# Attention slot order and TensorE wait placement in a fused attention and two-MLP kernel

## The chip, the core and the metric

The kernel runs on one core of a Trainium2 chip (trn2). The metric is the device time of one execution in microseconds, the median of three runs for the kernel before: 488.89 us (487.48 to 489.02). Engines are named as the profile names them: PE is TensorE (PEld its weight loads), DVE is VectorE, ACT is ScalarE, POOL is GpSimd, SP is the engine that issues the DMAs.

## The reference

Three stages follow one another: a local attention with block summaries, an MLP with a squared ReLU, and a second MLP whose hidden layer is a softmax-gated unit with a layer norm. Cut to what matters:

```python
# attention, B=2 H=8 S=768 D=64, block 32, window 16
k_sum = k.reshape(B, H, nb, block, D).max(axis=3)
v_sum = v.reshape(B, H, nb, block, D).mean(axis=3)
scores_l = where(|i - j| < window, scale * q @ k.T, -1e9)
scores_s = scale * q @ k_sum.T + log(block)
a = softmax(concat([scores_l, scores_s]))
x = a @ concat([v, v_sum])              # then (1536 tokens, 512)
# first MLP, 512 -> 2048 -> 512
h = maximum(x @ w_in, 0)
y = h * h @ w_out
# second MLP, 512 -> 1024 -> 512
h = y @ w_in
solu = h * softmax(h)
ln = (solu - mean(solu)) / sqrt(var(solu) + 1e-6) * g_ln
out = ln @ w_out
```

## The kernel before

Every large product is done in three matmuls, since each operand is split into a rounded part and the rest (`PASSES`: high x high, high x low, low x high). The attention is cut into 32 units `u`. A unit is a pair of heads and 192 query rows, three tiles of 64 rows, and has three parts on PE: `scores(u)` (L825, 64x64 tiles with 120 moving columns), `turned(u)` (L844, three transposes of the normalised probabilities) and `values(u)` (L874, 120 rows by 64 columns). Between scores and turned lie the eviction with mask and the maximum on DVE (`maxima`), the exponentials on ACT (`exps`) and the normalisation on DVE (`reciprocals`, `normalise`). Between turned and values ACT copies the result to SBUF (`copy_probsT`), and after values ACT makes `x_hi` (`x_high`) and DVE `x_lo` (`x_low`).

The first eight units run in the ramp. The other 24 are woven into the first MLP, which runs over four chunks of 384 tokens and 16 hidden tiles each: `up(n)` (L897, twelve 128x384 matmuls) and `down(n)` (L927, twelve more) alternate, two half steps per `n`. The table `SLOTS` says before which half step an attention slot stands and which units it handles: values of `a`, scores of `a + 2`, turned of `a + 1`. Slots are three half steps apart in the first chunk and four later. For units from 8 on, one PSUM bank pair serves all three: scores lie in bank 0, the transposed probabilities and the values' result in bank 1, where the result also reaches into the end of bank 0. `slot_ahead` puts waits that a coming slot needs on matmuls of the half step before it.

The second MLP goes over 12 tiles of 128 tokens. Step `s` on PE is: 24 matmuls of 512 columns for the hidden layer of tile `s` (L1022), eight transposes of the centred tile `s - 1` (L1037), and 24 matmuls for the output of tile `s - 2` (L1049). At `s = 0` and `s = 1` there is no output yet. On DVE a tile goes through its maximum (L774), `solu` (L782), `cen` (L789), and then the low part of the transposed tile before it, `lnT_lo` (L795). All engines run their own lists in the order of the code and meet at semaphores.

## Time and profile before

| what | before |
|---|---|
| median of three runs | 488.89 us (487.48 to 489.02) |
| the profiled execution | 488.89 us, its span 487.0 us |
| PE busy | 478.3 us, 98% of the span |
| DVE, ACT, POOL busy | 254.5, 207.6, 30.5 us |
| chain that ended last, by engine | PE 90%, DMA 3%, DVE 3%, SP 2%, ACT 1% |
| PE lines in the chain | L927 27%, L897 27%, L1049 12%, L1022 12%, L825 4%, L874 3%, L844 3%, L1037 2% |

The page gives one profiled execution. Its first part is the busy time of each engine; the chain is followed back from the last instruction to what released it, step by step. Matmuls are pipelined and their ends are modelled, so their records overlap: the distance between two starts is the time one took of the engine. A timeline row joins neighbouring instructions of one line, with the first start, the time from there to the last end, and their count. For values and scores each matmul has two records, so x12 stands for six. The granted clock is given as a share of full speed.

### The profile page before, as it was taken

What the parts mean: (1) busy time and instruction counts of PE and PEld (TensorE: products, weight loads), DVE (VectorE), ACT (ScalarE), POOL (GpSimd) and SP (SyncE); (2) the same over time, 40 slices, a digit from 0 to 9 for tenths busy, and PEclk for the clock granted to TensorE, in tenths of its full rate; (3) what the DMA queues carried; (4) which work ended last, traced back from release to release, by engine and by line L of the source; (5) the groups of instructions that cost most, each with busy time, mean ns of one, the idle gap of its engine ahead of it and who ended that gap; (6) DMA issues with size and microseconds to landing.
All of it is one profiled execution on the core that took longest, in us unless ns stands there. A gap on an engine that the chain in (4) does not pass through costs nothing.

```text
span 487.0 us, 8121 instructions
## 1 busy us (share of the span) xinstructions
PE 478.3 (98%) x3134; PEld 435.6 (89%) x3134; DVE 254.5 (52%) x511; ACT 207.6 (43%) x525; POOL 30.5 (6%) x62
## 2 busy tenths in 40 slices
PE   7899999999999999999999999999999999999997
PEld 5778999999999999999999999999888888888885
DVE  3779768886544444644443344446574444444440
ACT  2787665654343333533343333334353333333341
POOL 2421000211000000000000000000000000000000
PEclk9999999999999999999999999999999999999999
DMA  8999332121400010400000412121122000000001
GB/s 306 287 326 320 103 108 87 55 74 29 155 22 22 21 36 27 145 27 22 22 1 1 131 44 79 52 62 70 44 86 66 22 23 22 26 34 28 22 22 44
DMA packets 26823, 37.39 MB, mean 77 GB/s; under 512 B 2496, under 2 KB 16736, under 8 KB 26784
## 3 DMA queue, kind: packets, MB, share of 16 engines
q1 hardware_dynamic: 26784, 36.86, 24.2%
q8 instruction: 25, 0.41, 0.4%
q14 instruction: 14, 0.11, 0.1%
HBM read 30.41 MB, written 6.29 MB: 75 GB/s over the span
## 4 chain that ended last, share of the span: by engine, by line
PE 90%; DMA 3%; DVE 3%; SPq 2%; ACT 1%; issue 1%; ACTq 0%; DVEq 0%
PE bank L927 27%; PE bank L897 27%; PE bank L1049 12%; PE bank L1022 12%; PE bank L825 4%; DMA v_first<-vrows 3%; PE bank L874 3%; PE bank L844 3%; PE bank L1037 2%; DVE solu L782 1%; DVE stat L774 1%; DVE lnT_lo L795 0%; SPq L259 0%; SPq L250 0%; DVE cen L789 0%
## 5 line engine op out<-in xcount | busy, mean ns | idle before, releaser
L897 PE MATMUL bank<-x_hi,win_hi 128*128 128x384 f32 x256 | 87.9, 343 | 0.0
L927 PE MATMUL bank<-h_hi,wout_hi 128*128 128x384 f32 x256 | 86.0, 336 | 0.0
L897 PE MATMUL bank<-x_hi,win_lo 128*128 128x384 f32 x256 | 85.7, 335 | 0.0
L927 PE MATMUL bank<-h_hi,wout_lo 128*128 128x384 f32 x256 | 85.7, 335 | 0.0
L897 PE MATMUL bank<-x_lo,win_hi 128*128 128x384 f32 x256 | 85.7, 335 | 0.0
L927 PE MATMUL bank<-h_lo,wout_hi 128*128 128x384 f32 x256 | 85.6, 334 | 0.0
L651 DVE TENSOR_TENSOR sqr<-relu 128x384 f32<-128x384 f32 x64 | 35.9, 561 | 88.2 <-ACT relu L491 87.4
L491 ACT ACTIVATE relu<-bank 128x384 f32<-128x384 f32 x64 | 31.5, 491 | 108.9 <-PE bank L897 108.9
L897 PEld LDWEIGHTS bank<-x_hi,win_hi 128*128 128x128 f32 x256 | 48.1, 188 | 0.3 <-issue 0.2
L897 PEld LDWEIGHTS bank<-x_lo,win_hi 128*128 128x128 f32 x256 | 48.2, 188 | 0.0
L927 PEld LDWEIGHTS bank<-h_lo,wout_hi 128*128 128x128 f32 x256 | 48.1, 188 | 0.0
L927 PEld LDWEIGHTS bank<-h_hi,wout_hi 128*128 128x128 f32 x256 | 48.1, 188 | 0.0
L897 PEld LDWEIGHTS bank<-x_hi,win_lo 128*128 128x128 f32 x256 | 48.1, 188 | 0.0
L927 PEld LDWEIGHTS bank<-h_hi,wout_lo 128*128 128x128 f32 x256 | 48.1, 188 | 0.0
L774 DVE TENSOR_REDUCE stat<-bank 128x1 f32<-128x1024 f32 x12 | 14.7, 1225 | 49.1 <-PE bank L1022 49.1
L442 ACT ACTIVATE probs<-probs,neg_max 128x120 f32<-128x120 f32 x96 | 36.5, 382 | 8.7 <-DVE neg_max L624 8.6
L569 ACT ACTIVATE e_sb<-bank,stat 128x1024 f32<-128x1024 f32 x12 | 13.4, 1116 | 61.3 <-DVE stat L774 61.3
L1049 PE MATMUL bank<-win_hi,lnT_hi 128*128 128x512 f32 x96 | 38.4, 400 | 0.0
L655 DVE TENSOR_TENSOR h_lo<-sqr,h_hi 128x384 fp32r<-128x384 f32 x64 | 35.8, 559 | 4.3
L1049 PE MATMUL bank<-win_hi,lnT_lo 128*128 128x512 f32 x96 | 37.5, 391 | 0.0
L1049 PE MATMUL bank<-win_lo,lnT_hi 128*128 128x512 f32 x96 | 37.4, 390 | 0.0
L451 ACT COPY probsT<-bank 120x384 f32<-120x384 f32 x32 | 15.3, 478 | 48.0 <-PE bank L844 47.6
(79 smaller groups left out, 721.5 us busy)
## 6 DMA issues: line engine op xcount, KB each, us to landing
win_raw<-w_in_t SPq DMA_DIRECT2D x8, 512.0 KB, 12.8
wout_raw<-w_out_t SPq DMA_DIRECT2D x8, 512.0 KB, 14.1
win_raw<-w_t SPq DMA_DIRECT2D x8, 512.0 KB, 3.3
v_ext<-vwin SPq DMA_DIRECT2D x24, 144.0 KB, 3.2
k_raw<-kT SPq DMA_DIRECT2D x8, 400.0 KB, 4.1
out<-o_sb SPq DMA_DIRECT2D x12, 256.0 KB, 2.0
q_sb<-qT SPq DMA_DIRECT2D x24, 96.0 KB, 2.8
v_first<-vrows SPq DMA_DIRECT2D x4, 384.0 KB, 11.0
```

The lines of the kernel that those rows point to most:

```text
L442: last = nc.scalar.activation(probs[:, s, c], probs[:, s, c], ACT.Exp, bias=neg_max[:, s, t:t + 1], accum_out=row_sum[:, s, t:t + 1])
L451: nc.scalar.copy(probsT[0:KX, u % 2, :], src).then_inc(probsT_ok, 1)
L491: nc.scalar.activation(relu[:, n % 2, :], up_bank(n), ACT.Relu).then_inc(relu_ok, 1)
L651: nc.vector.tensor_tensor(sqr[:, n % 3, :], relu[:, n % 2, :], relu[:, n % 2, :], ALU.mult)\
L655: nc.vector.tensor_tensor(h_lo[:, n % 3, :], sqr[:, n % 3, :], h_hi[:, n % 3, :].bitcast(F32), ALU.subtract).then_inc(hlo_ok, 1)
L774: nc.vector.tensor_reduce(stat[:, p, 0:1], h2_bank(s), AX.X, ALU.max, negate=True).then_inc(m2_ok, 1)
L825: last = nc.tensor.matmul(out_[e * QT:(e + 1) * QT, t * KX:(t + 1) * KX], q_tile(u, rows, t), k_ext[rows, p, t * KX:(t + 1) * KX], start=T ...
L844: last = nc.tensor.transpose(turned_bank(u, t), probs[:, u % 2, t * KX:(t + 1) * KX], ident[:, 0:P])
L897: last = nc.tensor.matmul(up_bank(n), win[a][:, f * WC + k * P:f * WC + (k + 1) * P], x[b][:, c % 2, k * CH:(k + 1) * CH], start=(k == 0 a ...
L927: last = nc.tensor.matmul(down_bank(d), wout[a][:, f * WC + d * P:f * WC + (d + 1) * P], h[b][:, n % 3, :], start=(f == 0 and a == 0 and b ...
L1022: last = nc.tensor.matmul(bank[:, (0, 6)[p] + half, :], y_tile(s, a, k), w2[b][:, (k * FH + half) * WC:(k * FH + half + 1) * WC], start=(k ...
L1049: last = nc.tensor.matmul(bank[:, 4 + p, :], ln[a][:, p, f * P:(f + 1) * P], w2[b][:, (F2 + f) * WC:(F2 + f + 1) * WC], start=(f == 0 and ...
```

## The change

The change has two parts.

1. In a slot of the MLP loop, PE now issues values of `a`, then turned of `b`, then scores of `c`; scores and turned have changed places. PSUM is laid out anew for it: two of the transposed tiles lie in bank 1, the third in bank 0 behind the scores, and the values' result in bank 1 alone. ACT copies the transposed probabilities in two pieces, `copy_probsT` for two tiles and `copy_last` for the third, which waits until DVE has evicted the new scores. `x_high` loses its wait for that eviction and stands between the two copies. The wait for `q` moves from a matmul of the half step before to the second transpose.
2. In the second MLP, waits that stood in front of the transposes (L1037), of the output matmuls (L1049) and of the next hidden layer (L1022) now stand on matmuls in the middle of the stream before them. The waits for `cen`, `lnT_lo` and `o` are on the 16th, 19th and 22nd of the 24 matmuls of the hidden layer, those for `solu` and `y` on two of the last output matmuls.

```diff
@@ -213,12 +212,10 @@
         def turned_bank(u, t):
             if u < UPC:
                 return bank[0:KX, 1 + 2 * (u % 2), t * P:(t + 1) * P]
-            return bank[0:KX, 1, P + t * P:P + (t + 1) * P]
-
-        later_bank = bank[:, 0:2, :].rearrange("p b c -> p (b c)")
+            return bank[0:KX, 1, t * P:(t + 1) * P] if t < TPU - 1 else bank[0:KX, 0, UC:UC + P]
 
         def xT_bank(u):
-            return bank[:, 4 + u % 2, 0:UQ] if u < UPC else later_bank[:, WC - QT:WC - QT + UQ]
+            return bank[:, 4 + u % 2, 0:UQ] if u < UPC else bank[:, 1, 2 * P:2 * P + UQ]
 
         def mean_bank(p):
             return bank[0:NB, 6 + p % 2, 0:P]
@@ -447,15 +444,20 @@
                 act.wait_ge(probsT_ps, u + 1)
                 if u >= 2:
                     act.wait_ge(attn_ps, u - 1)
-                src = bank[0:KX, 1 + 2 * (u % 2), 0:TPU * P] if u < UPC else bank[0:KX, 1, P:P + TPU * P]
-                nc.scalar.copy(probsT[0:KX, u % 2, :], src).then_inc(probsT_ok, 1)
+                if u < UPC:
+                    nc.scalar.copy(probsT[0:KX, u % 2, :], bank[0:KX, 1 + 2 * (u % 2), 0:TPU * P])\
+                      .then_inc(probsT_ok, 1)
+                else:
+                    nc.scalar.copy(probsT[0:KX, u % 2, 0:2 * P], bank[0:KX, 1, 0:2 * P])
+
+            def copy_last(u):
+                act.wait_ge(masked_ok, min(u + 2, UNITS))
+                nc.scalar.copy(probsT[0:KX, u % 2, 2 * P:3 * P], turned_bank(u, 2)).then_inc(probsT_ok, 1)
 
             def x_high(u):
                 slot, cols = x_cols(u)
                 act.wait_ge(attn_ps, u + 1)
                 if u >= UPC:
-
-                    act.wait_ge(masked_ok, min(u + 3, UNITS))
                     act.wait_ge(probsT_ps, min(u + 2, UNITS))
                 if u >= 2 * UPC:
                     act.wait_ge(y_saved[u % PPB], 32 * (u // UPC - 1))
@@ -536,6 +538,7 @@
             hidden(1)
             copy_probsT(8)
             w_in_high(3)
+            copy_last(8)
             exps(9)
             w_out_high(1)
             for n in range(STEPS):
@@ -548,6 +551,8 @@
                         copy_probsT(SLOTS[h][1])
                     if h in X_AT:
                         x_high(X_AT[h])
+                    if h in SLOTS and SLOTS[h][1] is not None:
+                        copy_last(SLOTS[h][1])
                 for h in (2 * n, 2 * n + 1):
                     if h in SLOTS and SLOTS[h][2] is not None:
                         exps(SLOTS[h][2])
@@ -812,7 +817,7 @@
                     pe.wait_ge(qf_in[min(u, 2)], 16)
                 if u % UPB < PPB:
                     pe.wait_ge(kbc_ok, (u // UPB) * PPB + p + 1)
-                if u in (UPC, UPC + 1):
+                if u == UPC:
                     queries(u)
                 if 2 <= u <= UPC:
                     pe.wait_ge(masked_ok, u - 1)
@@ -841,6 +846,8 @@
                     pe.wait_ge(probsT_ok, u)
                 pe.wait_ge(norm_ok, u + 1)
                 for t in range(TPU):
+                    if t == 1 and UPC < u + 1 < UNITS:
+                        queries(u + 1)
                     last = nc.tensor.transpose(turned_bank(u, t), probs[:, u % 2, t * KX:(t + 1) * KX], ident[:, 0:P])
                 last.then_inc(probsT_ps, 1)
 
@@ -864,7 +871,6 @@
                         pe.wait_ge(xlo_ok, u - 1)
                 elif u == UPC:
                     pe.wait_ge(vkept_ok, 1)
-                    pe.wait_ge(masked_ok, UPC + 2)
                 elif UPB <= u < UPB + PPB:
                     pe.wait_ge(vs_in[p], 16)
                 pe.wait_ge(probsT_ok, u + 1)
@@ -880,9 +886,7 @@
             def slot_ahead(h, k):
 
                 if h + 1 in SLOTS:
-                    u, _, c = SLOTS[h + 1]
-                    if k == 1 and c is not None:
-                        queries(c)
+                    u = SLOTS[h + 1][0]
                     if k == 2:
                         pe.wait_ge(vw_in[u % PPB], 16 * (u // PPB - HPC + 1))
                     if k == 3:
@@ -982,10 +986,10 @@
                     if j in SLOTS:
                         a, b, c = SLOTS[j]
                         values(a)
+                        if b is not None:
+                            turned(b)
                         if c is not None:
                             scores(c)
-                        if b is not None:
-                            turned(b)
                     if j % 2 == 0:
                         up(n + 2)
                     else:
@@ -999,6 +1003,17 @@
                     return (y_hi, y_lo)[a][:, i % 2, k * P:(k + 1) * P]
                 at = k * CH + (i % TPC) * P
                 return x[a][:, (i // TPC) % 2, at:at + P]
+
+            def h2_ahead(s):
+
+                if s >= 2:
+                    pe.wait_ge(solu_ok, s - 1)
+
+            def y_ahead(s):
+                if s < (NCHUNK - 2) * TPC:
+                    pe.wait_ge(y_in[s % 2], 32 * (s // 2 + 1))
+                else:
+                    pe.wait_ge(yclo_ok, KD * (s // TPC + 1))
 
             for s in range(TT + 2):
                 p = s % 2
@@ -1010,14 +1025,18 @@
                         pe.wait_ge(xlo_ok, UNITS)
                     if s == 1:
                         pe.wait_ge(relu_ok, STEPS)
-                    if s >= 2:
-                        pe.wait_ge(solu_ok, s - 1)
-                    if s < (NCHUNK - 2) * TPC:
-                        pe.wait_ge(y_in[p], 32 * (s // 2 + 1))
-                    else:
-                        pe.wait_ge(yclo_ok, KD * (s // TPC + 1))
+                    if s < 3:
+                        h2_ahead(s)
+                        y_ahead(s)
                     for half in range(FH):
                         for k in range(KD):
+
+                            if half == 1 and k == 1 and s >= 2:
+                                pe.wait_ge(cen_ok, s)
+                            if half == 1 and k == 2 and s >= 2:
+                                pe.wait_ge(lnlo_ok, s - 1)
+                            if half == 1 and k == 3 and s >= 4:
+                                pe.wait_ge(o_ok, s - 3)
                             for a, b in PASSES:
                                 last = nc.tensor.matmul(bank[:, (0, 6)[p] + half, :], y_tile(s, a, k),
                                                         w2[b][:, (k * FH + half) * WC:(k * FH + half + 1) * WC],
@@ -1028,10 +1047,11 @@
                     down(STEPS - 2)
                     down(STEPS - 1)
                 if 1 <= s <= TT:
-                    pe.wait_ge(cen_ok, s)
                     if s == 1:
+                        pe.wait_ge(cen_ok, s)
                         pe.wait_ge(yclo_ok, KD * (NCHUNK - 1) + 2)
-                    else:
+                    elif s == TT:
+                        pe.wait_ge(cen_ok, s)
                         pe.wait_ge(lnlo_ok, s - 1)
                     for f in range(F2):
                         last = nc.tensor.transpose(bank[:, 2 + f // 4, (f % 4) * P:(f % 4 + 1) * P],
@@ -1041,10 +1061,16 @@
                     if s == 2:
                         pe.wait_ge(w2_lo_ok, F1)
                         pe.wait_ge(yclo_ok, KD * NCHUNK)
-                    if s >= 4:
+                    if s >= TT:
                         pe.wait_ge(o_ok, s - 3)
-                    pe.wait_ge(lnlo_ok, s - 1)
+                    if s == TT + 1:
+                        pe.wait_ge(lnlo_ok, s - 1)
                     for f in range(F2):
+
+                        if f == F2 - 2 and s + 1 < TT:
+                            h2_ahead(s + 1)
+                        if f == F2 - 1 and s + 1 < TT:
+                            y_ahead(s + 1)
                         for a, b in PASSES:
                             last = nc.tensor.matmul(bank[:, 4 + p, :], ln[a][:, p, f * P:(f + 1) * P],
                                                     w2[b][:, (F2 + f) * WC:(F2 + f + 1) * WC],
```

PE, a slot of the first chunk (unit 11 as `a`), before: values, scores, turned, and the first matmul of `down`.

```order
156 L874 MATMUL bank<-probsT,v_ext 64x64 [waits probsT_ok]
157 L874 MATMUL bank<-probsT,v_ext 64x64 x5
158 L825 MATMUL bank<-k_ext,q_sb 64x120 [waits kwin_ok]
159 L825 MATMUL bank<-k_ext,q_sb 64x120 x5
160 L844 MATMUL bank<-ident,probs 120x128 [waits norm_ok]
161 L844 MATMUL bank<-ident,probs 120x128 x2
162 L927 MATMUL bank<-h_hi,wout_hi 128x384 [waits hlo_ok,wout_lo_ok]
```

The same slot in the changed kernel, whose lines are numbered a little differently (L880 values, L851 turned, L830 scores, L931 down).

```order
158 L880 MATMUL bank<-probsT,v_ext 64x64 [waits probsT_ok]
159 L880 MATMUL bank<-probsT,v_ext 64x64 x5
160 L851 MATMUL bank<-ident,probs 120x128 [waits norm_ok]
161 L851 MATMUL bank<-ident,probs 120x128 [waits q_in3]
162 L851 MATMUL bank<-ident,probs 120x128
163 L830 MATMUL bank<-k_ext,q_sb 64x120 [waits kwin_ok]
164 L830 MATMUL bank<-k_ext,q_sb 64x120 x5
165 L931 MATMUL bank<-h_hi,wout_hi 128x384 [waits hlo_ok,wout_lo_ok]
```

The transposes now stand between values and scores, and scores stand next to the large matmuls.

PE, second MLP at `s = 2`, before: the last nine matmuls of the hidden layer and what follows them.

```order
1805 L1022 MATMUL bank<-win_hi,y_hi 128x512
1806 L1022 MATMUL bank<-win_lo,y_hi 128x512
1807 L1022 MATMUL bank<-win_hi,y_lo 128x512
1808 L1022 MATMUL bank<-win_hi,y_hi 128x512
1809 L1022 MATMUL bank<-win_lo,y_hi 128x512
1810 L1022 MATMUL bank<-win_hi,y_lo 128x512
1811 L1022 MATMUL bank<-win_hi,y_hi 128x512
1812 L1022 MATMUL bank<-win_lo,y_hi 128x512
1813 L1022 MATMUL bank<-win_hi,y_lo 128x512
1814 L1037 MATMUL bank<-ident,cen 128x128 [waits lnlo_ok,cen_ok]
1815 L1037 MATMUL bank<-ident,cen 128x128 x7
1816 L1049 MATMUL bank<-win_hi,lnT_hi 128x512 [waits lnlo_ok,yclo_ok,w2_lo_ok]
```

The same place in the changed kernel (L1041, L1057 and L1075 there).

```order
1828 L1041 MATMUL bank<-win_hi,y_hi 128x512 [waits cen_ok]
1829 L1041 MATMUL bank<-win_lo,y_hi 128x512
1830 L1041 MATMUL bank<-win_hi,y_lo 128x512
1831 L1041 MATMUL bank<-win_hi,y_hi 128x512 [waits lnlo_ok]
1832 L1041 MATMUL bank<-win_lo,y_hi 128x512
1833 L1041 MATMUL bank<-win_hi,y_lo 128x512
1834 L1041 MATMUL bank<-win_hi,y_hi 128x512
1835 L1041 MATMUL bank<-win_lo,y_hi 128x512
1836 L1041 MATMUL bank<-win_hi,y_lo 128x512
1837 L1057 MATMUL bank<-ident,cen 128x128 x8
1838 L1075 MATMUL bank<-win_hi,lnT_hi 128x512 [waits yclo_ok,w2_lo_ok]
```

The two waits of the transposes have moved nine and six matmuls ahead.

## Rows read from the trace of the kernel before

**Rows 1.** The page: span, PE's busy time, the chain's shares by engine.
```profile
span 487.0 us, 8121 instructions
...
PE 478.3 (98%) x3134; PEld 435.6 (89%) x3134; DVE 254.5 (52%) x511; ACT 207.6 (43%) x525; POOL 30.5 (6%) x62
...
PE 90%; DMA 3%; DVE 3%; SPq 2%; ACT 1%; issue 1%; ACTq 0%; DVEq 0%
```

**Rows 2.** Stretches: length, busy of each engine, PEclk, DMA share, GB/s.
```profile
105.00:280.00 175.00, 175.00 (x1265) 167.68 (x1264) 83.10 (x176) 68.91 (x201) 7.09 (x16) 1.00 0.15 46
```

**Rows 3.** Waits of PE, the longest: total us, times, longest us.
```profile
PE bank L825 <- DMA q_first<-q_head: 1.7, 1, 1.7
```

**Rows 4.** Timeline of PE, a slot of the first chunk: start, us, instruction.
```profile
67.22 0.57 PE L874 MATMUL bank<-probsT,v_ext 120*64 120x64 f32 x12
67.72 0.83 PE L825 MATMUL bank<-k_ext,q_sb 64*64 64x120 f32 x12
68.48 0.54 PE L844 MATMUL bank<-ident,probs 128*120 128x128 f32 x3
68.78 0.42 PE L927 MATMUL bank<-h_hi,wout_hi 128*128 128x384 f32 x1
69.04 0.34 PE L927 MATMUL bank<-h_lo,wout_hi 128*128 128x384 f32 x1
```

**Rows 5.** Timeline of PE, the last two slots, which have no scores.
```profile
260.60 0.57 PE L874 MATMUL bank<-probsT,v_ext 120*64 120x64 f32 x12
261.10 0.54 PE L844 MATMUL bank<-ident,probs 128*120 128x128 f32 x3
...
270.42 0.45 PE L897 MATMUL bank<-x_hi,win_hi 128*128 128x384 f32 x1
270.70 0.34 PE L897 MATMUL bank<-x_lo,win_hi 128*128 128x384 f32 x1
```

**Rows 6.** Timeline of PE in the ramp: transposes, then scores.
```profile
23.30 0.55 PE L844 MATMUL bank<-ident,probs 128*120 128x128 f32 x3
23.78 0.83 PE L825 MATMUL bank<-k_ext,q_first 64*64 64x120 f32 x12
```

**Rows 7.** Timeline of PE, the one place where scores stand before large matmuls.
```profile
38.12 0.83 PE L825 MATMUL bank<-k_ext,q_sb 64*64 64x120 f32 x12
38.88 0.44 PE L897 MATMUL bank<-x_hi,win_hi 128*128 128x384 f32 x1
39.16 0.33 PE L897 MATMUL bank<-x_lo,win_hi 128*128 128x384 f32 x1
```

**Rows 8.** Timeline of PE's weight loads at the same place.
```profile
38.88 0.19 PEld L897 LDWEIGHTS bank<-x_hi,win_hi 128*128 128x128 f32 x1 [0.16 <-issue]
```

**Rows 9.** The chain: twelve matmuls behind scores, and twelve behind transposes.
```profile
38.95 2.30 PE bank L897 x12
...
45.07 2.09 PE bank L897 x12
```

**Rows 10.** Timelines of DVE and PE: the tightest normalisation, and the next slot.
```profile
98.23 0.53 DVE L638 TENSOR_TENSOR probs<-probs,row_rec 128x360 f32<-128x360 f32 x1
...
99.17 0.57 PE L874 MATMUL bank<-probsT,v_ext 120*64 120x64 f32 x12
```

**Rows 11.** Timelines of DVE and of weight loads behind the slot of unit 23.
```profile
192.71 0.36 DVE L644 TENSOR_TENSOR x_lo<-bank,x_hi 128x192 fp32r<-128x192 f32 x1
...
193.17 0.19 PEld L897 LDWEIGHTS bank<-x_hi,win_hi 128*128 128x128 f32 x1
```

**Rows 12.** The chain in the second MLP: an output block and a hidden block.
```profile
371.75 5.49 PE bank L1049 x24
377.24 5.44 PE bank L1022 x24
```

**Rows 13.** The chain at s = 2: the low part on DVE, then the transposes.
```profile
357.60 1.14 DVE lnT_lo L795
...
358.88 1.06 PE bank L1037 x8
```

**Rows 14.** Timeline of PE at s = 2: the 19th matmul of the hidden layer.
```profile
357.21 0.39 PE L1022 MATMUL bank<-win_hi,y_hi 128*128 128x512 f32 x1
```

## The prediction, made before the changed kernel ran

> **What bounds the kernel now.** I read the page first: TensorE (PE) is busy 98% of the span and holds 90% of the chain that ended last [rows 1], with the granted clock at 1.00, the 2.4 GHz level [rows 2]. PE's waits come next: the longest is 1.7 us, in the ramp [rows 3]. From about 40 us to 465 us PE does its list without a pause, so a change pays only through the distance from one matmul start to the next. The views that matter are therefore PE's own timeline, read start to start (its durations are modelled and overlap), and the chain. I call the attention matmuls of a slot V (values, L874), S (scores, L825) and T (transposes, L844), and F the 128x384 matmuls of the up and down steps around them.
>
> **Part 1: the slot order, V S T to V T S.** Of the 24 slots in the MLP loop 22 have all three parts; the last two have no scores. In such a slot now V starts at 67.22, S at 67.72, T at 68.48, F at 68.78, the second F at 69.04 [rows 4]: 0.50 + 0.76 + 0.30 + 0.26 = 1.82 us. The third step is the telling one: F starts 0.30 after three transposes began, as if they were part of its stream, while every other pair of neighbours pays a gap. The new order is put together from rows that hold the same neighbours: V to T 0.50 (260.60 to 261.10) [rows 5]; T to S 0.48 (23.30 to 23.78) [rows 6]; S to F 0.76 (38.12 to 38.88) and F to its second 0.28 (to 39.16) [rows 7]. Sum 2.02 us, +0.20 per slot. What happens: S has 64x64 tiles, V 120x64, T and F the whole array or nearly so; V S T F changes the shape three times and V T S F four times. The weight load of the first F behind S comes after 0.16 of idle time [rows 8], where in the stream a load is hidden. The chain says the same in its own way: the F block behind S is 2.30 us, that behind T 2.09 [rows 9]. 22 x 0.20 = +4.4 us, all of it on the path.
>
> The bounds. There is one S-to-F place in the trace, and its first F has two waits. Lowest: the second F comes 0.17 after the first, as in the stream, instead of 0.28: 0.20 - 0.11 = 0.09, 2.0 us. Highest: the starts behind the second F are uneven too, as the 2.30 of rows 9 allows, 0.04 more: 0.24, 5.3 us. I stay with 0.20, since each of its four terms is a row of the very pair.
>
> The Trainium skill, "TensorEngine Tiling (Array Packing)", Key Properties, says that changing the tiling mode drains TensorE; it gives no price, and by its count the new order has one drain more in each slot, so it speaks against this part of the change, as rows 7 do. The Trainium skill, "TensorE: Matmul & The Clock Gate", The mechanism, says that a weight load which meets no conflict is pulled ahead of matmuls in flight. By that the first load behind S would be hidden and the part would cost its lower bound, 2.0 us; rows 8 show that it was not pulled ahead there.
>
> **What moves beside it, at nothing.** The wait for q goes from a step of F to the second transpose, later than before, on data asked for two slots earlier. The copy of the transposed probabilities becomes two ACT copies, the second behind the eviction of the new scores; they are needed only at the next slot, 6 us or more later. T comes 0.76 earlier in its slot and needs the normalised probabilities there: at the tightest slot they end at 98.76, V starts at 99.17 and so T at 99.67 [rows 10], 0.9 us of room. DVE starts on new scores 0.48 later than now, so 0.4 us or more is left. The x copy on ACT loses its wait for the scores' eviction; no engine waits for it but at one place.
>
> That place is the third chunk's start (unit 23), whose x_lo is needed by the last quarter of the F block right behind its slot. Now x_lo runs from 192.71 to 193.07 and the load that needs it starts at 193.17 [rows 11]. DVE evicts S first, and S ends 0.48 later; x_lo then ends near 193.5, while PE wants it at 193.17 + 0.20. With the restart +0.2 us (0 to 0.4).
>
> **Part 2: the waits of the second MLP are moved forward.** Each now stands alone on a matmul of a stream. For s = 3 to 11 a tile's cen and lnT_lo are done before that stream begins, so the moved waits never hold. What they could give back is the slower stretch behind the transposes: an L1049 block takes 5.49 us where the same 24 matmuls of L1022 take 5.44 [rows 12]. Nine tiles x 0 to 0.05: -0.2 us (0 to -0.45).
>
> For s = 2 it is another matter. Here the pipeline fills, and now PE reaches the transposes early and is held until 358.88 by lnT_lo, which DVE begins at 357.60, when cen has ended, and ends at 358.74 [rows 13]. The waits for cen and lnT_lo move in front of the 16th and the 19th of the 24 matmuls of L1022. The 19th now starts at 357.21 [rows 14], the 16th three starts of 0.227 (5.44 / 24) earlier, at 356.53. Work that needs neither tile is put behind them: PE stalls about 1.1 us at the first, runs three matmuls, stalls again until about 358.8, and still has six matmuls to do before the transposes. 6 x 0.227 = 1.36, and the first start after a pause is some 0.08 slower. They begin near 360.3, and all behind them shifts: +1.4 us (1.3 to 1.5). Behind PE the reduction of the same tile on DVE and everything after it shifts alike, so nothing else is late next. The ramp, and the tail behind the last tile, keep their order.
>
> **Sum.** The profiled execution is 488.89 us with a span of 487.0 [rows 1]; 1.9 us lie around it and stay. It is also the median of the three runs. 4.4 + 0.2 - 0.2 + 1.4 = +5.8; 488.9 + 5.8 = **494.7 us**.
>
> **The rivals.**
> (a) The order costs half: the row behind S is slow for its two waits, not for the change of shape. For it: it is the only such place. Against: the F behind V alone, with one wait, has 0.28 to its second too (270.42 to 270.70) [rows 5]. Slots +2.0: 488.9 + 2.0 + 0.2 - 0.2 + 1.4 = 492.3. 10%.
> (b) A new wait in the slots: normalised probabilities come too late for the earlier T, because ACT's second copy waits for DVE and holds the exponentials. It decides if they come more than 0.9 us later than now at the tightest slot; I see half of that. If four of the crowded slots of the first chunk lose 0.5 each, +2.0: 496.7. 8%.
> (c) The moved waits do not hold PE at s = 2. It needs cen and lnT_lo of that tile over 1 us earlier than now. Against: the DVE chain in front of them starts from the end of L1022 of s = 1, which is not touched. 494.7 - 1.4 = 493.3. 5%.
> (d) Faster than before: the new order saves changes of shape instead of adding one, since V and T both have 120 rows. Against: V to T costs the same 0.50 as V to S [rows 4, 5]. If V T flowed as T F does, some 0.2 less, the slots would come out even: 490.3. With the gap behind S gone as well (0.11) they would gain 22 x 0.11 = 2.4: 487.9; to show as faster they must gain (1.5 + 1.4) / 22 = 0.13 a slot or more, 487.4. 2%.
> The forecast has 75%.
>
> **How the numbers follow.** The forecast's own bounds and runs of the same kernel, which spread from 487.48 to 489.02, make 492.0 to 496.4; that takes in (a) and (c) and leaves out (b), (d) and the far ends, under 2 in 10. A difference under 0.3%, 1.5 us, can't be told from none. The forecast, (a), (b) and (c) are slower by more, 98%, from which I take one for what is not listed; within 2%, faster 1%.
>
> **What would show it.** In the slots: the second F 2.02 us behind V, F blocks of 2.3 in the chain behind S, the load of the first F behind 0.16 of idle time. 1.91 or less would prove (a). At s = 2: two pauses inside the L1022 stream with cen and lnT_lo as releasers, and the transposes 1.4 us later, counted from the start of that stream. At unit 23: a short pause before the 10th F. In (b) T would show idle time released by the normalisation. The forecast is wrong as a whole if PE has pauses of its own elsewhere, or if slots cost as much as now.

## The result, and the profile after

| | before | after |
|---|---|---|
| median | 487.89 us (485.85 to 489.02, six runs) | 492.01 us (491.73 to 493.78, six runs) |
| ratio, with its 95% interval | | 1.0094 (1.0067 to 1.0121) |
| the profiled execution | 488.89 us, span 487.0 | 493.14 us, span 491.3 |
| start of the first large block behind the slots' first scores (the ramp) | 38.88 us | 37.22 us |
| from there to the end of the span (the body) | 448.1 us | 454.1 us |

The changed kernel is slower by 0.9%, 4.1 us between the medians. The last two rows are the ones to work with. The ramp ends where PE starts its first large matmul behind the scores of the first slot. Up to there both kernels wait for their first loads; from there PE works almost without a pause. The body grew by 5.9 us: the two profiled executions are 4.25 us apart, and the ramp of this one execution happened to be 1.66 us shorter.

The page of the changed kernel: span, busy time of the engines, shares of the chain by engine and by line. It answers to [rows 1].

```profile
span 491.3 us, 8100 instructions
...
PE 480.5 (98%) x3134; PEld 434.1 (88%) x3134; DVE 253.1 (52%) x511; ACT 210.5 (43%) x549; POOL 30.7 (6%) x62
...
PE 91%; DMA 3%; DVE 3%; SPq 1%; ACT 1%; issue 1%; ACTq 0%; DVEq 0%
```

PE is still 98% busy with the same 3134 matmul records, and its busy time grew by 2.2 us only. Apart from the span, nothing in this page tells a reader that the body lost 6 us, or where. The time at a change of shape shows in the distances between starts, not in the busy time.

The slot of the first chunk that answers to [rows 4], in PE's timeline of the changed kernel, with the last large matmul ahead of it (start, us, instruction):

```profile
65.91 0.34 PE L901 MATMUL bank<-x_hi,win_lo 128*128 128x384 f32 x1
66.17 0.57 PE L880 MATMUL bank<-probsT,v_ext 120*64 120x64 f32 x12
66.67 0.54 PE L851 MATMUL bank<-ident,probs 128*120 128x128 f32 x3
67.15 0.83 PE L830 MATMUL bank<-k_ext,q_sb 64*64 64x120 f32 x12
67.91 0.45 PE L931 MATMUL bank<-h_hi,wout_hi 128*128 128x384 f32 x1
68.19 0.34 PE L931 MATMUL bank<-h_lo,wout_hi 128*128 128x384 f32 x1
```

V to T 0.50, T to S 0.48, S to F 0.76, F to its second 0.28: 2.02 us, against 1.82 in [rows 4]. The same slot in the weight loads of the changed kernel, at the step from scores to F:

```profile
67.91 0.19 PEld L931 LDWEIGHTS bank<-h_hi,wout_hi 128*128 128x128 f32 x1 [0.16 <-issue]
```

The load of F comes after idle time, as in [rows 8]; it was not pulled ahead.

The chain of the changed kernel, one slot and the twelve matmuls behind it (start, us, what), answers to [rows 9]:

```profile
49.86 0.50 PE bank L880 x12
...
51.59 2.31 PE bank L931 x12
...
59.80 2.28 PE bank L901 x12
```

The large block behind the scores takes 2.28 or 2.31 us, where the block behind the transposes took 2.09. From one such block to the next it is 59.80 - 51.59 = 8.21 us.

PE's timeline of the changed kernel in the hidden layer of s = 2, which answers to [rows 13, 14]:

```profile
355.91 0.48 PE L1041 MATMUL bank<-win_hi,y_hi 128*128 128x512 f32 x1
...
360.53 0.50 PE L1041 MATMUL bank<-win_hi,y_hi 128*128 128x512 f32 x1 [0.96 <-DVE cen L794]
...
361.66 0.50 PE L1041 MATMUL bank<-win_hi,y_hi 128*128 128x512 f32 x1 [0.17 <-DVE lnT_lo L800]
...
363.18 1.03 PE L1057 MATMUL bank<-ident,cen 128*128 128x128 f32 x8
```

Two pauses inside the stream, released by cen and by lnT_lo. From the stream's start to the transposes it is 363.18 - 355.91 = 7.27 us. In before the stream starts at 353.04 and the transposes at 358.88: 5.84. So +1.43.

The waits of PE in the changed kernel, the longest (total us, times, longest us):

```profile
PE bank L860 <- DMA v_first<-vrows: 1.9, 2, 1.4
PE bank L830 <- DMA q_first<-q_head: 1.7, 2, 1.1
PE bank L940 <- POOL idle L393: 1.1, 1, 1.1
PE bank L1041 <- DVE cen L794: 1.0, 1, 1.0
PE bank L851 <- DVE probs L643: 0.8, 3, 0.3
PE bank L1041 <- DVE lnT_lo L800: 0.2, 1, 0.2
```

All of these but the two at L1041 lie in the ramp. Besides them the body has one wait, of 0.2 us for lnT_lo in front of the last transposes, and before has the same one there. No slot of the body has a wait in it.

### The profile page after: what moved, and what is told of

Same layout as the page of the kernel before. It is cut to its first block, busy times and chain, and to the rows that moved or that the text cites. A ratio compares the mean times of both kernels' runs of the same rounds, so it can differ in the third digit from the quotient of the medians.

```text
span 491.3 us, 8100 instructions
## 1 busy us (share of the span) xinstructions
PE 480.5 (98%) x3134; PEld 434.1 (88%) x3134; DVE 253.1 (52%) x511; ACT 210.5 (43%) x549; POOL 30.7 (6%) x62
## 4 chain that ended last, share of the span: by engine, by line
PE 91%; DMA 3%; DVE 3%; SPq 1%; ACT 1%; issue 1%; ACTq 0%; DVEq 0%
PE bank L901 28%; PE bank L931 27%; PE bank L1041 13%; PE bank L1075 12%; PE bank L830 4%; DMA v_first<-vrows 3%; PE bank L880 3%; PE bank L851 3%; PE bank L1057 2%; DVE solu L787 1%; DVE stat L779 1%; DVE lnT_lo L800 0%; SPq L247 0%; SPq L256 0%; DVE cen L794 0%
## 5 line engine op out<-in xcount | busy, mean ns | idle before, releaser
L931 PE MATMUL bank<-h_hi,wout_hi 128*128 128x384 f32 x256 | 86.0, 336 | 0.0
L931 PE MATMUL bank<-h_hi,wout_lo 128*128 128x384 f32 x256 | 85.6, 335 | 0.0
L931 PE MATMUL bank<-h_lo,wout_hi 128*128 128x384 f32 x256 | 85.6, 334 | 0.0
L931 PEld LDWEIGHTS bank<-h_hi,wout_hi 128*128 128x128 f32 x256 | 48.0, 188 | 0.7 <-issue 0.5
L931 PEld LDWEIGHTS bank<-h_lo,wout_hi 128*128 128x128 f32 x256 | 48.0, 188 | 0.0
L931 PEld LDWEIGHTS bank<-h_hi,wout_lo 128*128 128x128 f32 x256 | 48.1, 188 | 0.0
L1075 PE MATMUL bank<-win_hi,lnT_hi 128*128 128x512 f32 x96 | 38.4, 400 | 0.0
L1075 PE MATMUL bank<-win_hi,lnT_lo 128*128 128x512 f32 x96 | 37.5, 390 | 0.0
L1075 PE MATMUL bank<-win_lo,lnT_hi 128*128 128x512 f32 x96 | 37.4, 389 | 0.0
L497 ACT ACTIVATE h_hi<-relu 128x384 fp32r<-128x384 f32 x64 | 33.7, 527 | 2.0
```

The source lines that it names most:

```text
L497: nc.scalar.activation(h_hi[:, n % 3, :], relu[:, n % 2, :], ACT.Square).then_inc(hhi_ok, 1)
L931: last = nc.tensor.matmul(down_bank(d), wout[a][:, f * WC + d * P:f * WC + (d + 1) * P], h[b][:, n % 3, :], start=(f == 0 and a == 0 and b ...
L1075: last = nc.tensor.matmul(bank[:, 4 + p, :], ln[a][:, p, f * P:(f + 1) * P], w2[b][:, (F2 + f) * WC:(F2 + f + 1) * WC], start=(f == 0 and ...
```

## The experiments

**How they are compared.** The ramps of these executions lie up to 5.2 us apart, so each kernel's profile is read as ramp and body, defined as above. All these kernels compute everything that before computes. Times and ratios are this kernel over before on the same chip.

| kernel | median, and before beside it | ratio (95%) | ramp | body |
|---|---|---|---|---|
| before | 487.89 | | 38.88 | 448.1 |
| e7_before_again (profiled only, 488.09) | | | 38.24 | 448.1 |
| e12_before_third (profiled only, 487.95) | | | 38.03 | 448.1 |
| after | 492.01, 487.89 | 1.0094 (1.0067 to 1.0121) | 37.22 | 454.1 |
| e8_after_again (profiled only, 493.33) | | | 37.43 | 454.0 |
| e11_after_timed | 492.71, 486.82 | 1.0119 (1.0085 to 1.0153) | 39.35 | 454.0 |
| e1_order_only | 490.77, 486.57 | 1.0083 (1.0057 to 1.0110) | 34.16 | 452.6 |
| e2_waits_only | 487.36, 486.57 | 1.0022 (1.0004 to 1.0041) | 36.92 | 449.5 |
| e3_waits_from3 | 486.87, 486.57 | 1.0007 (0.9987 to 1.0026) | 35.95 | 448.1 |
| e4_turned_first | 487.51, 486.57 | 1.0022 (0.9998 to 1.0046) | 36.08 | 449.6 |
| e5_full_scores | 493.94, 487.01 | 1.0141 (1.0117 to 1.0164) | 38.41 | 452.9 |
| e6_full_scores_order | 490.46, 487.01 | 1.0067 (1.0034 to 1.0101) | 35.41 | 454.2 |
| e9_full2_order | 485.67, 486.96 | 0.9971 (0.9946 to 0.9995) | 36.71 | 447.1 |
| e10_full2_scores | 485.21, 486.96 | 0.9963 (0.9939 to 0.9987) | 37.41 | 447.2 |

**e1_order_only: the slot order alone.** The part of the change in the MLP loop; the second MLP has the waits of before.

```diff
-                        if c is not None:
-                            scores(c)
...
+                        if c is not None:
+                            scores(c)
...
-                    u, _, c = SLOTS[h + 1]
-                    if k == 1 and c is not None:
-                        queries(c)
+                    u = SLOTS[h + 1][0]
...
+                    if t == 1 and UPC < u + 1 < UNITS:
+                        queries(u + 1)
```

> Part 1 of the change alone: values, turned, scores with its PSUM layout and the split ACT copy; the second MLP's waits as before. I read the body, the time from the first large matmul behind scores in the ramp (38.88 before, 37.22 after) to the end of the span: 448.1 us before, 454.1 after. Theory (the order costs, by one more change of array shape a slot): a slot 0.19 to 0.22 longer, 22 slots, body about 452.6 (+4.4 to +4.6). Rival (the second MLP's stall carries most of the +4.1 us of the medians): body under 451. On the ramp: if the 1.7 us shorter ramp of the changed kernel is a matter of this execution's DMA, the ramp here lies anywhere between 37.2 and 38.9; if the layout or the order caused it, it is 37.2 again.

Body 452.6 against 448.1: +4.5 us. 22 slots at 0.20 make 4.4, and the profile has 8.18 to 8.21 from slot to slot in the first chunk where before has 7.99. This is the larger part of the change, and rival (a), half of it, is refuted. The ramp, 34.16, lies below the range of 37.2 to 38.9 that was expected for it.

**e2_waits_only: the second MLP alone.** Slot order of before.

```diff
+                            if half == 1 and k == 1 and s >= 2:
+                                pe.wait_ge(cen_ok, s)
+                            if half == 1 and k == 2 and s >= 2:
+                                pe.wait_ge(lnlo_ok, s - 1)
```

> Part 2 alone: the moved waits of the second MLP on the kernel before. Theory: PE pauses inside the hidden layer's stream at s = 2 and the transposes there start 1.4 us later; nothing is given back elsewhere; body 449.5 (+1.4). Rival (moved waits give back around the transposes what they lose at s = 2): body 448.1 to 448.6. On the ramp: chance says anything between 37.2 and 38.9, a cause in part 1 says 38.9.

Body 449.5: +1.4 us. PE waits for cen and lnT_lo as in the changed kernel, 1.0 and 0.2 us, with the stream-to-transposes distance at s = 2 being 358.31 - 351.07 = 7.24 us, 1.40 more than before's 5.84.

**e3_waits_from3: the same, but s = 2 as before.** Only the one tile at which the moved waits hold PE goes back.

```diff
-                            if half == 1 and k == 1 and s >= 2:
+                            if half == 1 and k == 1 and s >= 3:
...
-                            if half == 1 and k == 2 and s >= 2:
+                            if half == 1 and k == 2 and s >= 3:
...
-                    elif s == TT:
+                    elif s in (2, TT):
```

> Part 2 alone with the waits for cen and lnT_lo moved only from s = 3 on; at s = 2 they stand in front of the transposes as before. Theory: the whole price of part 2 was that one place, so the body is 448.1 within 0.1, and the transposes at s = 2 start where they did. Rival (moved waits gain, 0.05 a tile): body 447.7. If moved waits cost by themselves, body over 448.3.

Body 448.1, the same as before's to a tenth, and the distance at s = 2 is 5.84 again (350.09 to 355.93). So the whole price of part 2 is the stall at s = 2, and the moved waits of the other tiles neither cost nor give back anything. The prediction had put 0.2 us back there.

**e4_turned_first: T V S.** The transposes first, then values, then scores. It puts T next to F on the other side and has as many changes of shape as before (F T flows, then V, S, F), while S still stands in front of F. On e1, with the copy of the transposed probabilities bound to the place of the new order:

```diff
-                    act.wait_ge(attn_ps, u - 1)
+                    act.wait_ge(attn_ps, u if u > UPC else u - 1)
...
+                    if k == 1:
+                        pe.wait_ge(probsT_ok, u + 1)
...
-                        values(a)
...
+                        values(a)
```

> Part 1 with the order turned, values, scores: scores stand next to the large matmuls as in the changed kernel, but the transposes stand next to the large matmuls too, so the array changes its shape three times a slot, not four. Second MLP as before. Shape theory: a slot costs what it did before or up to 0.06 more, body 448.0 to 449.5. Rival (what costs is scores in front of large matmuls, whatever the count): 0.2 more a slot, body 452.5, as in the run with the order alone.

Its slot in PE's timeline:

```profile
64.35 0.34 PE L903 MATMUL bank<-x_hi,win_lo 128*128 128x384 f32 x1
64.53 0.49 PE L851 MATMUL bank<-ident,probs 128*120 128x128 f32 x3
64.94 0.57 PE L880 MATMUL bank<-probsT,v_ext 120*64 120x64 f32 x12
65.44 0.83 PE L830 MATMUL bank<-k_ext,q_sb 64*64 64x120 f32 x12
66.20 0.44 PE L933 MATMUL bank<-h_hi,wout_hi 128*128 128x384 f32 x1
66.48 0.34 PE L933 MATMUL bank<-h_lo,wout_hi 128*128 128x384 f32 x1
```

T starts 0.18 behind a large matmul, within 0.01 of the large matmuls' own distance: no gap. S to F is 0.76 and F to its second 0.28, as in the changed kernel. From the last large matmul to the second one behind the slot it is 66.48 - 64.35 = 2.13 us. The changed kernel has 68.19 - 65.91 = 2.28 with the same S in front of F. Before has 2.09: its row ahead of [rows 4] is

```profile
66.95 0.34 PE L897 MATMUL bank<-x_hi,win_lo 128*128 128x384 f32 x1
```

So what costs is not that scores stand in front of F; it is the fourth change of shape. The new PSUM layout and the split copy are those of e1, so they are not what costs either. The body is 1.5 us longer than before's, a tenth above the range that was expected. The chain shows where it lies. From one large block behind scores to the next in the first chunk it is 58.23 - 50.17 = 8.06 us:

```profile
50.17 2.30 PE bank L933 x12
...
58.23 2.30 PE bank L903 x12
```

Before has 7.99 there, and in the second chunk it is 10.13 against 10.07. So a slot costs 0.06 to 0.07 more than before, of which 0.04 lie between the two rows compared above and the rest further on in the large blocks; 22 slots make 1.3 to 1.5 us.

**e5_full_scores and e6_full_scores_order: scores on the whole array.** If the change of shape is what costs, scores of the shape of their neighbours should be indifferent to the order. The queries are laid out with zeros on the off-diagonal blocks, so that three 128x128 matmuls do what six of 64x64 did: same products, plus zeros. e5 has the order V S' T, e6 has V T S'. Against before (e5):

```diff
-        q_sb = sb(att, "q_sb", [P, PPB, UQ], F32)
+        q_sb = sb(att, "q_sb", [P, QR, 2 * UQ], F32)
...
+                    if u >= UPC:
+                        last = nc.tensor.matmul(out_[:, t * KX:(t + 1) * KX], q_tile(u, None, t),
+                                                k_ext[:, p, t * KX:(t + 1) * KX],
+                                                start=True, stop=True, skip_group_check=True)
+                        continue
...
+            sp.wait_ge(scores_ok, UPC + 1)
+            load_q(UPC + QR)
```

> The kernel before, its order values, scores, turned, with the scores of units 8 and on done as three full-array matmuls against block-diagonal queries (zeros in the other head's corners) in place of six 64x64 ones; the queries lie in a ring of three buffers. Same moving columns, so the stream of the scores stays 0.57 to 0.62 us; the array changes its shape twice a slot (into values, out of values), not three times. Shape theory: the pause and the slow first transpose between scores and turned go, 0.1 to 0.2 us a slot, 22 slots, body 443.7 to 446 (before 448.15). Rival (what costs is a gap each block brings with it, whatever the shape, or full-array weight loads that can't be hidden behind 120 columns): body 448 or more.

> Part 1 of the change (values, turned, scores) with the same full-array scores. Shape theory: with scores of the same shape as their neighbours it is the same two changes in either order, so the body equals that of the other order within 0.5 us: the 4.5 us of the order are gone. Rival (scores in front of large matmuls cost by themselves, whatever their shape): 0.2 a slot stay, the body is 4.4 above that of the other order.

Neither gave what it was made for, and by an accident of mine. The wider buffer has room for three units (QR = 3), so the load of the fourth, unit 11, was issued only after the first scores of the slots, behind the weights in the queue. The waits of PE, e5 and then e6:

```profile
PE bank L912 <- DMA q_sb<-qT: 3.9, 1, 3.9
```

```profile
PE bank L866 <- DMA q_sb<-qT: 4.8, 1, 4.8
```

The stalls alone do not make up the bodies. Stretches of e5 (bounds, length, busy time of PE, PEld, DVE, ACT, POOL, granted clock, DMA share, GB/s):

```profile
48.00:52.00 4.00, 1.21 (x7) 0.88 (x6) 2.57 (x6) 1.91 (x8) 0.00 (x0) 1.00 1.02 278
52.00:56.00 4.00, 2.86 (x21) 2.42 (x21) 0.03 (x1) 0.52 (x2) 0.00 (x0) 0.79 0.09 23
56.00:60.00 4.00, 4.00 (x27) 3.88 (x24) 2.50 (x5) 2.21 (x8) 0.43 (x1) 0.78 0.40 84
```

PE resumes at 53.14. Its large matmuls start 0.17 or 0.18 apart up to 54.30 and about 0.3 apart right after that, so the clock fell a little over 1 us after the pause had ended. It was below full speed for (0.21 + 0.22) x 4 = 1.7 us' worth. 3.9 + 1.7 = 5.6, and 452.9 less 5.6 is 447.3. That is still above the 443.7 to 446 expected for e5: the scores on the whole array give back less per slot than I had thought. The same sum for e6: from 53.33, where its pause ends, to about 58.4 its large matmuls start 0.32 apart instead of 0.17, so about half of 5.1, 2.5 us, are lost; 4.8 + 2.5 = 7.3, and 454.2 less 7.3 is 446.9. The next pair takes the stall away to measure this directly; its expectations, 446.8 and 447.1, were worked out from the undisturbed slots of e5 and e6.

**e9_full2_order and e10_full2_scores: the same without the stall.** Unit 11 gets a buffer of its own and the six small matmuls; the ring of three skips it. Everything else is as in e6 (V T S') and e5 (V S' T).

```diff
+        q_odd = sb(att, "q_odd", [P, UQ], F32)
...
+                if u == ODD:
+                    sp.dma_start(q_odd[:, :], qT[u, :, :]).then_inc(qo_in, 16)
+                    return
...
-                    if u >= UPC:
+                    if u >= UPC and u != ODD:
```

> As e6 (values, turned, scores with full-array scores), but unit 11's queries keep a buffer and the six 64x64 matmuls of their own, so that its load no longer waits for a free buffer in the ring; second MLP as before. In the undisturbed slots of e6 a slot was 3.66 us against 3.73 before, in those of e5 3.69. Shape theory with that stall gone: body 448.1 - 21 x 0.07 + 0.2 = 446.8, 1.3 us under the kernel before; the medians about 1.3 us (0.3%) lower. Rival (full-array scores cost elsewhere): body over 448.

> As e5 (values, scores, turned with full-array scores), unit 11 as in e9. Shape theory: body 448.1 - 21 x 0.045 = 447.1; the difference between the two orders, 5.9 and 4.5 us with 64x64 scores, is here under 0.5 us and has the other sign. Rival: the order with the scores next to the large matmuls is 4 us longer here too.

Bodies 447.1 and 447.2: the two orders, 4.5 us apart with small scores, are even. PE's timeline of e9, a slot:

```profile
64.81 0.34 PE L929 MATMUL bank<-x_hi,win_lo 128*128 128x384 f32 x1
65.08 0.57 PE L908 MATMUL bank<-probsT,v_ext 120*64 120x64 f32 x12
65.58 0.54 PE L879 MATMUL bank<-ident,probs 128*120 128x128 f32 x3
65.96 0.83 PE L849 MATMUL bank<-k_ext,q_sb 128*128 128x120 f32 x6
66.55 0.42 PE L959 MATMUL bank<-h_hi,wout_hi 128*128 128x384 f32 x1
66.81 0.34 PE L959 MATMUL bank<-h_lo,wout_hi 128*128 128x384 f32 x1
```

and its weight loads at the step from scores to F:

```profile
65.85 0.75 PEld L849 LDWEIGHTS bank<-k_ext,q_sb 128*128 128x128 f32 x6
66.52 0.19 PEld L959 LDWEIGHTS bank<-h_hi,wout_hi 128*128 128x128 f32 x1
```

Here the load of F has no idle time in front of it and starts before its matmul, if only by 0.03, at 66.52 for 66.55; behind the 64x64 scores of [rows 8] it came after 0.16 of idle time and started with its matmul, both at 38.88. T to S' is 0.38 where T to S was 0.48. From the last large matmul to the second behind the slot e9 has 2.00, e10 has 2.03, each with two changes of shape; before has 2.09 with three, the changed kernel 2.28 with four.

Both are faster than before, by 0.3% and 0.4% with intervals that end below 1. The best version that was run is e10, 0.9963 (0.9939 to 0.9987). The chains agree in size. From one scores step to the next in the second chunk, e10:

```profile
128.56 0.86 PE bank L844 x6
...
138.58 0.86 PE bank L844 x6
```

10.02 us (and 10.00 in e9, 128.29 to 138.29). Before has 10.07 there:

```profile
131.54 2.09 PE bank L897 x12
...
141.61 2.09 PE bank L897 x12
```

21 slots x 0.05 is 1.05 us for e10 (measured 0.9); in its chain the first large block of the second chunk takes 2.22 where before has 2.11, which is the rest. For e9 21 x 0.07 is 1.5, of which its one slot with small scores gives 0.2 back. The chain shows two more places that give some back: the slot of unit 23 is 10.14 long where its neighbours have 10.00, and the first large block of the second chunk takes 2.18 for 2.11. That leaves 1.1, for 1.0 measured. Why that first block is longer was not looked into.

**e7, e8, e11, e12: the two kernels again, unchanged.** They were run to learn how much of a difference lies in the execution and how much in the kernel.

> The kernel before, once more, for its ramp and its body. If the ramp is a matter of chance (arrival of the first loads), the body is 448.15 within 0.1 and the ramp somewhere between 34 and 39 us, the range of the five kernels so far; if the changed layout shortens the ramp, it is 38.9 within 0.3.

> The changed kernel once more, for its ramp and its body: body 454.06 within 0.1. Chance: ramp anywhere between 34 and 39 us; a cause in the change: 37.2 within 0.3.

> The changed kernel, timed again against the kernel before, to see where 1.8 us of the 5.9 us by which its body is longer went in the medians (492.01 against 487.89). Theory (ramps vary by chance, and the first comparison drew long ramps for the kernel before): the ratio here is 1.009 to 1.014, near the 1.012 of the bodies. Rival (the changed kernel's ramp is shorter by its layout): the ratio stays at 1.008 or below.

> A third profile of the kernel before, for the ramp: chance says anything between 34 and 39 us, with a body of 448.1; a ramp that belongs to the kernel says 38.2 to 38.9.

Three executions of before have bodies of 448.1, and three of the changed kernel 454.1, 454.0 and 454.0. The body is the same to 0.1 us; the ramps lie between 34.16 and 39.35 over all the kernels. Taken alone, e8's ramp of 37.43 fits a ramp that the change has made shorter as well as it fits chance. Against the first stand e2 and e3, which lack part 1 of the change and have 36.92 and 35.95, and e11, the same kernel as e8 with 39.35. For the first two profiles, before and then the changed kernel, the chain shows what made the difference:

```profile
9.01 16.21 DMA v_first<-vrows
```

```profile
8.32 15.25 DMA v_first<-vrows
```

This one load lands at 25.22 in one and at 23.57 in the other, and that is 1.65 of the 1.66 us between their two ramps. It does not explain every ramp. In e11 the load lands at 24.22, 1.0 us before that of before, yet the ramp is 0.5 us longer: the granted clock was 0.57 from 24 to 28 us, half of full speed for most of that stretch, and the twelve matmuls that waited for the load took 2.71 us instead of 1.50. In e1 and e8 this load does not stand in the chain at all.

## Why the prediction was right, point by point

**Slots, +0.20 each.** Right to the hundredth. The 2.02 us from V to the second F were put together from four steps of before, and all four steps came out as they stood in those rows: 0.50, 0.48, 0.76, 0.28. e1's body says +4.5 for +4.4. The doubt that made the bounds, whether the one S-to-F place in the ramp was slow for its waits, is settled: the slots of the body and of e4 have the same 0.76 and 0.28, and the chain has 2.28 to 2.32 for every block behind scores, with no wait of PE among them.

**The reason given.** I counted changes of shape, three against four. e4 holds the place of S in front of F and takes one change away, and the slot falls from 2.28 to 2.13. e9 takes away two and falls to 2.00. Order as such, with all else equal, is worth nothing once the scores have the shape of their neighbours (e9 against e10). The count is a good rule but not a price: the steps are uneven, 0.06 to 0.13 from two changes to three and 0.15 to 0.19 from three to four, and from two to three the scores' own work is another one too.

The Trainium skill, "TensorEngine Tiling (Array Packing)", Key Properties, says that a change of tiling mode drains TensorE. The traces agree in that every further change of shape made the slot longer, and they add the price here: 0.15 to 0.2 us for the fourth in a slot. The Trainium skill, "TensorE: Matmul & The Clock Gate", The mechanism, has a load pulled ahead of matmuls in flight when nothing conflicts. Behind 64x64 scores it never was, in any slot of the changed kernel that was looked at (0.16 idle each); behind scores of the whole array no time is idle and the load starts 0.03 before its matmul (e9), where inside a stream of large matmuls the next one's load starts 0.17 before it. Had that rule held across the shapes, part 1 would have cost 2.0 us; it cost 4.5.

**What moves beside it, at nothing.** Right. The waits of PE show none in a slot. The body of e1 leaves 0.1 for all of it together.

**Unit 23, +0.2.** The step was missized: it cost next to nothing. The row of x_lo in DVE's timeline of the changed kernel, and those of PE at the 10th matmul of the block:

```profile
194.40 0.35 DVE L649 TENSOR_TENSOR x_lo<-bank,x_hi 128x192 fp32r<-128x192 f32 x1
```

```profile
193.27 0.45 PE L901 MATMUL bank<-x_hi,win_hi 128*128 128x384 f32 x1
...
194.97 0.34 PE L901 MATMUL bank<-x_hi,win_hi 128*128 128x384 f32 x1
```

x_lo ends at 194.75, 0.22 before the 10th matmul starts. The nine distances up to that matmul are 1.70 us, and the whole block is 2.32 against 2.28 or 2.31 for the others. I had let x_lo end 0.1 to 0.2 after it was wanted and added a restart of PE; it was just in time. The mechanism itself is real, as e9 shows: there x_lo of that unit ends at 190.34, the 10th matmul starts at 190.39 with 0.27 to the one behind it, and the block takes 2.24 for the 2.11 or 2.12 of the others.

**s = 2, +1.4.** Right: +1.43 in the changed kernel, +1.40 alone in e2, gone in e3. Rival (c) is refuted. The first pause was put at about 1.1 and was 0.96. The second was forecast to end at about 358.8, which is 5.76 us behind the stream's start in before; it ended 5.75 behind it (361.66 less 355.91). The six matmuls behind it were the price, as said.

**The moved waits of the other tiles, -0.2.** Wrong, nothing came back. In the chain of the changed kernel the first two output blocks are:

```profile
364.21 5.49 PE bank L1075 x24
...
376.02 5.45 PE bank L1075 x24
```

The first output block still takes 5.49 as in [rows 12], without a wait between the transposes and it; the next takes 5.45. Further on both kernels have blocks of 5.46 and of 5.48 or 5.49 in turn. So the slower stretch of [rows 12] was not the waits' doing. e3's body, equal to before's, closes the point.

**The sum and the time.** +4.4 + 0.2 - 0.2 + 1.4 = +5.8 was forecast for the body, and e1's +4.5 with e2's +1.4 make +5.9, the changed kernel itself +5.9 to +6.0. Yet the median came out at 492.0 and not 494.7, on the lower edge of the range. The step that failed is the base. The sum was made on the profiled execution, 488.89, which was also the median of three; with three more runs before's median is 487.89, so 1.0 of the 2.7 us is there. The other 1.7 us are the forecast 5.8 less the 4.1 between the medians. They cannot be in the body if the timed runs are like the profiled ones, whose body repeats to 0.1. The timed difference was 4.1 us in one set of runs and 5.9 in the other (e11: 492.71 against 486.82), on a difference of bodies that never moved, and e11's ratio of 1.0119 is what the bodies give: 5.9 / 488 = 1.2%. So the 1.7 would be in the ramps of those runs. That is argued and not shown, and no cause is needed for it beyond the spread of the runs: the interval of the first comparison, 1.0067 to 1.0121, has the 1.2% in it. That the median came to lie inside the range, by 0.01 us, is luck, and the time alone would have misled. It lies nearest to the 492.3 of rival (a), which e1 refutes; only the body shows that the mechanism was the forecast one.

**Rivals.** (a) refuted by e1; (b) refuted, there is no wait of T in any slot of the body; (c) refuted by e2; (d) refuted, V to T costs 0.50, as its row said.

## What to carry to other kernels

When the bounding engine is full, a change of instruction order is priced by putting the new sequence together from starts in the old trace that have the same neighbours, even if a pair stands there only once; busy shares show none of it. Group small matmuls so that those of one shape stand together, or give them the shape of their neighbours by padding with zeros, and a wait that is moved forward and is not met yet costs not its own length but all that stands behind it and did not need it; one that is met costs nothing (e3). Before a forecast is tied to one execution's time, split that time into the stretch that waits for the first loads and the rest: here the rest repeats to 0.1 us in three profiled executions of each kernel, and the first stretch wanders by several.

## What the runs showed that was not expected

- In both runs with a long pause of PE the granted clock fell, and it stayed low while PE was at work again. In e5 a pause of 3.9 us was followed by clocks of 0.79 and 0.78 over 8 us, a mixture of the 2.4 and the 1.2 GHz level, and cost 1.7 us more. The fall came when PE had been back at work for over 1 us. In e6, with a pause of 4.8 us, the clock was at the lower level before the pause had ended (0.50 from 52 to 53 us); about 5.1 us of matmuls ran at it (128x384 matmuls 0.32 apart instead of 0.17), which cost 2.5 more. In these two runs the late load cost about one and a half times its wait.
- The clock takes part in the spread of the timed runs too. Of the 74 timed executions of before that stand beside the experiments, nine have a mean granted clock of 0.997 or less. Their median is 488.9 us, and that of the other 65 is 486.7.
- Full-array scores behind values take longer to the next step than behind transposes: 0.77 us in e10, 0.59 in e9, for the same three matmuls. The step behind them differs too (transposes in e10, F in e9), so which neighbour does it is not shown. In e10 transposes to F is then 0.25, and the two slots come out nearly even, 2.03 and 2.00.

```profile
66.14 0.93 PE L844 MATMUL bank<-k_ext,q_sb 128*128 128x120 f32 x6
66.91 0.49 PE L872 MATMUL bank<-ident,probs 128*120 128x128 f32 x3
67.16 0.42 PE L955 MATMUL bank<-h_hi,wout_hi 128*128 128x384 f32 x1
```
